# Exact exponentials of an attention kernel in a ring of three SBUF buffers instead of PSUM

## The reference

```python
def _attn_ref(q, k, v):
    B, H, S, D = q.shape                                   # 4, 8, 1152, 64
    scale = 1.0 / np.sqrt(D)
    q_pool = q.reshape(B, H, S // 2, 2, D).mean(axis=3)
    scores = scale * np.matmul(q_pool, k.transpose(0, 1, 3, 2))
    scores = scores - np.max(scores, axis=-1, keepdims=True)
    attn = np.exp(scores)
    attn = attn / (np.sum(attn, axis=-1, keepdims=True) + 1e-09)
    return np.matmul(attn, v).astype(np.float32)

def _moe_ref(x, w_in, w_out):                              # 512 -> 2048 -> 512
    h = x @ w_in
    return ((h * (1.0 / (1.0 + np.exp(-h)))) @ w_out).astype(np.float32)

def _moe2_ref(x, w1, w2, w3, w_out):                       # 512 -> 1024 -> 512
    return (((x @ w1) * (x @ w2)) @ w3 @ w_out).astype(np.float32)
```

## Time and profile before

| what | value |
|---|---|
| median of 3 runs | 1292.55 us (1292.16 to 1293.73) |
| the profiled execution | 1292.74 us, its span 1291.0 us |
| instructions | 26235 |
| TensorE busy | 1279.6 us, 99% |
| VectorE / ScalarE / GpSimd busy | 604.9 / 588.9 / 364.6 us |
| granted clock of TensorE | 1.00 |

### The profile page before, as it was taken

One profiled execution on the slowest core, in us unless ns is written; L12 is line 12 of the kernel. 1 busy time (PEld: TensorE's weight loads), 2 busy tenths in 40 slices (PEclk: granted clock), 3 DMA queues, 4 the chain that ended last, 5 costly groups with the idle time before them and its releaser, 6 DMA issues.

```text
span 1291.0 us, 26235 instructions
## 1 busy us (share of the span) xinstructions
PE 1279.6 (99%) x10980; PEld 1152.0 (89%) x10980; DVE 604.9 (47%) x904; ACT 588.9 (46%) x1081; POOL 364.6 (28%) x312
## 2 busy tenths in 40 slices
PE   8999999999999999999999999999999999999999
PEld 6999999999999999888888888888988888888888
DVE  6788788888887878443212111111156222222222
ACT  3777777777777776743322222222245212121111
POOL 4566766666666666510000000000000000000000
PEclk9999999999999999999999999999999999999999
DMA  4222222222222211021000000001052000000001
GB/s 141 66 69 64 71 75 74 75 74 75 75 74 74 75 56 38 20 67 49 17 1 1 1 1 1 1 1 49 2 180 98 1 1 34 1 33 1 33 5 46
DMA packets 26007, 58.60 MB, mean 45 GB/s; under 512 B 7200, under 2 KB 8736, under 8 KB 25888
## 3 DMA queue, kind: packets, MB, share of 16 engines
q1 hardware_dynamic: 25888, 56.91, 13.9%
HBM read 52.04 MB, written 4.79 MB: 44 GB/s over the span
## 4 chain that ended last, share of the span: by engine, by line
PE 97%; DVE 1%; POOL 0%; DMA 0%; issue 0%; ACT 0%; SPq 0%; POOLq 0%; DVEq 0%; ACTq 0%
PE psum L945 19%; PE psum L946 19%; PE psum L947 19%; PE psum L1021 18%; PE psum L962 10%; PE psum L998 9%; PE psum L1000 3%; DVE mx L734 1%; PE psum L973 1%; DMA kraw<-in_kT 0%; POOL pL L464 0%; POOL kL L450 0%; ACT pH L554 0%; PE psum L1031 0%; POOL qsum L492 0%
## 5 line engine op out<-in xcount | busy, mean ns | idle before, releaser
L734 DVE TENSOR_REDUCE mx<-psum 128x2 f32<-128x768 f32 x240 | 228.5, 957 | 72.0 <-PE psum L962 69.8
L554 ACT ACTIVATE pH<-psum 128x576 fp32r<-128x576 f32 x288 | 187.9, 653 | 145.6 <-PE psum L1000 142.7
L464 POOL TENSOR_TENSOR pL<-pF,pH 128x576 fp32r<-128x576 f32 x111 | 158.3, 1426 | 148.2 <-ACT pF L561 148.1
L876 DVE TENSOR_TENSOR gL<-gF,gH 128x512 fp32r<-128x512 f32 (+1 forms) x80 | 52.2, 653 | 310.3 <-ACT gH L636 310.3
L1021 PE MATMUL psum<-pH,vH 64*128 64x288 f32 x1152 | 187.9, 297 | 1.9 <-POOL pL L464 0.9
L1021 PE MATMUL psum<-pH,vL 64*128 64x288 f32 x1152 | 185.6, 292 | 0.0
L1021 PE MATMUL psum<-pL,vH 64*128 64x288 f32 x1152 | 185.4, 292 | 0.0
L633 ACT ACTIVATE gF<-psum 128x512 f32<-128x512 f32 (+1 forms) x80 | 44.4, 556 | 269.8 <-PE psum L947 269.8
L768 DVE TENSOR_TENSOR pL<-psum,pH 128x576 fp32r<-128x576 f32 x177 | 132.8, 750 | 35.1 <-ACT psum L563 35.1
L1021 PEld LDWEIGHTS psum<-pH,vH 64*128 64x128 f32 x1152 | 123.5, 185 | 4.4 <-POOL pL L464 1.6
L1021 PEld LDWEIGHTS psum<-pH,vL 64*128 64x128 f32 x1152 | 123.9, 185 | 0.0
(11 more groups left out here) (104 smaller groups left out, 2799.0 us busy)
## 6 DMA issues: line engine op xcount, KB each, us to landing
vraw<-in_v SPq DMA_DIRECT2D x16, 576.0 KB, 4.6
qraw<-in_qT SPq DMA_DIRECT2D x15, 576.0 KB, 5.0
kraw<-in_kT SPq DMA_DIRECT2D x15, 576.0 KB, 3.8
rsums<-recips SPq DMA_DIRECT2D x32, 144.0 KB, 3.1
wstage<-in_w_in SPq DMA_DIRECT2D x16, 256.0 KB, 4.6
fstage<-in_w3T SPq DMA_DIRECT2D x8, 512.0 KB, 4.7
w12stage<-in_w SPq DMA_DIRECT2D x8, 512.0 KB, 4.7
outT<-oS SPq DMA_DIRECT2D x4, 1024.0 KB, 4.2
```

The source lines that it names most:

```text
L464: pool.tensor_tensor(pL[r][:], pF[pool_order(n) % 2][:], pH[r][:].bitcast(F32), ALU.subtract).then_inc(pL_pool, 1)
L554: act.activation(pH[r][:], scores, ACT.Exp, scale=SCALE).then_inc(pH_ready, 1)
L734: dve.tensor_reduce(mx[:, qt, :, kb], bank[:, :, 0:KW], AX.X, ALU.max).then_inc(max_taken, 1)
L876: dve.tensor_tensor(gL[r][:, w], gF[:, w], gH[r][:, w].bitcast(F32), ALU.subtract).then_inc(gL_ready, 1)
```

## The change

`pF` becomes a ring of three buffers, used by all units: the exact exponential of unit n goes to `pF[n % 3]` and never back into `stbank`. VectorE's `p_lo` takes its first input from there. ScalarE waits, ahead of the exact exponential of n, for the low part of n - 3. TensorE's transposed scores of unit n wait for the exact exponential of n - 2, for every unit, where they waited for the low part of n - 2 for units of VectorE.

```diff
--- before.py
+++ after.py
@@ -112,7 +112,7 @@
             mrow = [sb(f"mrow{j}", [Q], F32R, st) for j in range(2)]
             vH = sb("vH", [NC, 3, D], F32R, st)
             vL = sb("vL", [NC, 3, D], F32R, st)
-            pF = [sb(f"pF{r}", [2, HALF], F32, st) for r in range(2)]
+            pF = [sb(f"pF{r}", [2, HALF], F32, st) for r in range(3)]
             pH = [sb(f"pH{r}", [2, HALF], F32R, st) for r in range(RING)]
             pL = [sb(f"pL{r}", [2, HALF], F32R, st) for r in range(RING)]
             mx = sb("mx", [QT, 2, KB], F32, st)
@@ -461,7 +461,7 @@
                 pool.wait_ge(pH_ready, n + 1)
                 need(pool, pv_done, 2 * (n - RING + 1))
                 r = n % RING
-                pool.tensor_tensor(pL[r][:], pF[pool_order(n) % 2][:], pH[r][:].bitcast(F32), ALU.subtract
+                pool.tensor_tensor(pL[r][:], pF[n % 3][:], pH[r][:].bitcast(F32), ALU.subtract
                                    ).then_inc(pL_pool, 1)
 
             def w_lo(i):
@@ -556,11 +556,9 @@
                     place_even(between)
                 if n % NC == 1 and n > NC:
                     take_o((n - NC) // UNITS, (n - NC) // NC % 2)
-                if by_pool(n):
-                    need(act, pL_pool, pool_order(n) - 1)
-                    act.activation(pF[pool_order(n) % 2][:], scores, ACT.Exp, scale=SCALE).then_inc(pF_ready, 1)
-                else:
-                    act.activation(scores, scores, ACT.Exp, scale=SCALE).then_inc(pF_ready, 1)
+                if n >= 3:
+                    act.wait_ge(*lo_done(n - 3))
+                act.activation(pF[n % 3][:], scores, ACT.Exp, scale=SCALE).then_inc(pF_ready, 1)
 
             def place_even(p):
 
@@ -765,7 +763,7 @@
                 dve.wait_ge(pF_ready, n + 1)
                 dve.wait_ge(pH_ready, n + 1)
                 need(dve, pv_done, 2 * (n - RING + 1))
-                dve.tensor_tensor(pL[r][:], stbank[n % 2], pH[r][:].bitcast(F32), ALU.subtract).then_inc(pL_dve, 1)
+                dve.tensor_tensor(pL[r][:], pF[n % 3][:], pH[r][:].bitcast(F32), ALU.subtract).then_inc(pL_dve, 1)
 
             def w_hi(i):
                 dve.wait_ge(wstage_loaded, 16 * (i + 1))
@@ -988,7 +986,7 @@
                     pe.wait_ge(m_placed_even, 2 * (p + 1))
                     pe.wait_ge(m_placed_odd, p + 1)
                 if n >= 2:
-                    pe.wait_ge(*((pF_ready, n - 1) if by_pool(n - 2) else lo_done(n - 2)))
+                    pe.wait_ge(pF_ready, n - 1)
                 keys, q = slice(c * P, (c + 1) * P), qhalf(a)
                 out = stbank[n % 2]
                 for s, (k, r) in enumerate(((kH, qH), (kL, qH), (kH, qL))):
```

## The result

The changed kernel takes 1348.93 us (median, 1348.46 to 1349.39), the kernel before 1292.22 us in the same comparison: a ratio of 1.0433, 95% interval 1.0423 to 1.0444, or 56.7 us more. Forecast were 1329 us, with a range of 1303 to 1356.

The account below looks back on a forecast made before the run. The bound was the slackless ring of TensorE's score block and VectorE's maximum. Holds of 37 us, less 0.2 for TensorE's wait, plus 0.5 for longer subtractions, on 1292.5 gave 1329 us, range 1303 to 1356.

Parts of the forecast that it names:

- TensorE's wait: Transposed scores of unit n wait for ScalarE's exponential of n-2, not the subtraction: 0.2 us gained, at most 1 us.
- ScalarE's wait: ScalarE's exact exponential of n waits for the low part of n-3; by program order it costs nothing.
- ScalarE's writes: 177 exponentials go to SBUF instead of PSUM, 654 ns for 651 each: nothing.
- The hold: VectorE's two-SBUF-input subtractions wait for a running GpSimd instruction and end 0.61 us after it.
- The sum over the holds of subtractions: Holds of VectorE's eleven subtractions laid over one old pair: 2.45 us a pair, 15 pairs, 37 us.
- the first item: VectorE's subtraction at 268.76, held by GpSimd's q sum until 270.17: next maximum 1.02 us late.
- The third: VectorE's subtraction at 281.38, held by GpSimd's normalizing product until 282.51: 0.68 us.
- GpSimd held by VectorE ... I take zero: Subtractions block GpSimd instructions up to 0.6 us, mostly hidden in its idle time: zero, up to 1 us a pair.
- Clock ... I take no change: TensorE's granted clock stays at 1.00, 2.4 GHz, though stalls make it idle 7% of the attention stage.
- no hold: Rival: VectorE's subtraction isn't held beside GpSimd and stays at 0.75 us; 1292 to 1294 us; chance 0.10.
- phases settle: Rival: VectorE's subtractions slide into GpSimd's idle time; 0.75 us a pair remain, 11 us, 1304 us; chance 0.13.
- the two engines fill up: Rival: held GpSimd work also stalls TensorE, 1 to 2 us a pair; 68 us and more, 1360; chance 0.12.

Follow-up runs that it names:

- the run with another order: Changed kernel with GpSimd's low part of k between its subtractions of units 15 and 16, not ahead of both: 1322.54 us, ratio 1.0228.
- 1316: Changed kernel with the reduced maxima (mcol) in unused columns of a PSUM bank: 1316.39 us, ratio 1.0179.
- 1308 us: Changed kernel with the maxima in PSUM and GpSimd's sum of q behind its subtraction of unit 7: 1307.68 us, ratio 1.0112.
- 1325: Kernel before, with VectorE's subtraction taking its first input from a constant tile of zeros in SBUF: 1325.33 us, ratio 1.0246.
- 1334: Changed kernel with GpSimd's low part of k behind its subtractions of units 15 and 16: 1333.56 us, ratio 1.0311.
- 1324 us: Changed kernel with maxima in PSUM, q's sum behind unit 7's subtraction, k's low part behind the subtractions of units 15 and 16: 1323.95 us, ratio 1.0238.
- the first two experiments: Changed kernel with VectorE's subtraction reading PSUM: 1292.73 us; kernel before with only that subtraction's first input moved to SBUF zeros: 1325.33 us.

## Where the prediction was right, and where its size came out by luck

**TensorE's wait, ScalarE's wait, ScalarE's writes: right.** With all of the change but the second SBUF input the time is 1292.73 us, and a fourth buffer changes nothing. ScalarE's two kinds of writes, 651 and 654 ns, are 653 ns for all. The waits in the trace have none of ScalarE for a subtraction. VectorE's own length stayed at 750 ns in the median, where 755 were forecast; it didn't get shorter either.

**The hold: right in kind.** 0.60 to 0.63 us from the end of GpSimd's instruction to that of the held subtraction, against the forecast 0.61; the longest is 2.02 us, near 2 as forecast, the mean 0.99 for about 1.1. The rule of the Trainium skill (SBUF — State Buffer, Who interferes with whom) covers it: two SBUF inputs on VectorE against GpSimd's reads. The trace of the changed kernel agrees, and so does the run whose only edit is that input (1017 ns in the mean for 750). Of the two kinds of instruction that the prediction counted as agreeing with that rule, only the negation has two SBUF inputs; the cast has one and shows only that it is held.

**The sum over the holds of subtractions: too large, 37 us for 23.** With the negation out of the way the loss is 1316.4 - 1293.2 = 23.2 us, 1.5 us a pair instead of 2.45 (in the trace a steady pair takes 34.95 us there for 33.25, which is 1.7); the low bound that I gave was 21. In the list, the first item was right in kind (the subtraction beside the sum of q ends 1.95 us after its start, 1.20 later than unheld; taking it away gave 8.7 us, 0.6 a pair, not 1.02). The third, 0.68 us, did not come: VectorE's subtraction of 270.71 started 0.02 us ahead of the normalizing product, and GpSimd was held. In its place the subtraction of unit 14 (274.62) was held 0.98 us, because GpSimd's subtraction of unit 13 ran late. And the cast of `w_hi`, 1062 ns in the median before, is mostly free in the changed kernel (498 ns in the mean). A list taken from the old timeline gives the size of such holds, not which instruction will be held.

**The step that failed: "GpSimd held by VectorE ... I take zero".** I looked for who waits for GpSimd's late results. What I didn't ask is what VectorE instruction a late GpSimd meets. Before, GpSimd's subtraction of unit 15 ran from 286.76 to 288.18 and the next began at 288.62, so the negation of 287.84 waited 0.2 us and found the gap. Holds of GpSimd ahead of them, about 1 us in all, closed that gap: the two ran back to back, and the negation, on TensorE's path, was held for 2.3 us in each of 13 pairs. (Back to back alone is not enough for so long a hold, as the run with another order shows.) TensorE waits 24.4 us for it, 0.9 of them in the first pair as before, so its cost is 23.5 us.

**The step "Clock ... I take no change": wrong.** The prediction named a lower clock among the signs of being wrong, and it came. Six pairs at the lower level for 3.4 us took 38.2 and not 36.8 us: 6 x 1.44 = 9 us. In the steady part it came only behind stalls of TensorE of 1.8 us: where those are gone (1316, 1322 and 1308 us, and 1325, 1334 and 1324 us) there is none. At the start it is otherwise: near 28 us the profiled executions of the changed kernel, of the one with a ring of four, of the one with the maxima in PSUM and of the one that subtracts from PSUM have one such stretch, behind an idle time of about 1.15 us that the kernel before has too, without it. The stretch from 500 to 552 of the earlier trace rows, with an idle share of 3.5%, was a poor witness, since its idle time came in short pieces (0.3 us at most).

Together: 23 for the subtractions, 23.5 for the negation and 9 for the clock are 55.5 of the 56.7 us; the rest is about what the medians of the kernel before differ by from one comparison to the other (1292.2 and 1293.2). The negation and its clock are the 32.5 us of one run; their split is read from the trace. The pair took 36.8 or 38.2 us and not 35.7. That the measured time lay in the range was luck: the first term was 14 us too high while two terms were missing. The term that I had, rightly sized, would have given 1316 us. Of the rivals, "no hold" is refuted by the first two experiments; "phases settle" is half true (the low bound of the subtractions); "the two engines fill up" came near in its size, but through the negation and not by TensorE waiting at L1019 for GpSimd's low parts, which is 1.6 us.

**Left open.** Why the negation lost to GpSimd's second subtraction in the changed kernel, each of 13 times, and won in the run with one SBUF input added to the kernel before and in the one with another order, with GpSimd's next instruction equally close behind. Neither the length of the instruction nor how early GpSimd's next is released tells the cases apart. Open too is why only six of the thirteen equal stalls were followed by the lower clock. What still costs 15 us in the kernel of 1307.68 us was seen in its timeline only (units 11 to 14 and 0 to 3) and not taken apart by runs.

## What to carry to other kernels

Ahead of moving an input of a VectorE instruction from PSUM to SBUF, count its SBUF inputs. With two of them it and the GpSimd instructions beside it, all of which read SBUF here, held each other up; with one it was never held (745 to 759 ns). What the move frees in PSUM has to be worth that. Look in the trace for a two-input instruction with a long maximum, and price the holds on both engines: a delayed instruction meets others that were safe before by a gap of half a microsecond. A short two-input instruction on the critical path can be freed of the holds by putting one small input into PSUM (2.3 us became 0.16, and the kernel 32.5 us faster).

## What the runs showed of the hardware

- A held VectorE subtraction of 576 columns ends 0.60 to 0.63 us after GpSimd's instruction (66 of them), where a free one takes 0.75: some 0.14 us of its start is spent inside the hold.
- A held VectorE subtraction came between two GpSimd instructions, and the second is recorded 0.5 us longer (q's low part 1.32 us for 0.81). A negation of 10 columns lost that turn in 13 of 13 cases in the changed kernel and waited for a second instruction of 1.4 us too (2.3 us for 0.16 of work), and got it in 13 of 13 in two other kernels (0.95 us).
- With starts 0.02 us apart the earlier instruction ran free and the later was held (VectorE at 270.71 took 0.74 us, GpSimd at 270.73 took 2.02 for 1.43).
- A subtraction with both inputs in SBUF and one with an input in PSUM take the same 750 ns at 576 columns.
- After six of thirteen stalls of 1.8 us TensorE was granted 1.2 GHz for about 3.4 us, which cost 1.44 us each. After the stalls of 0.9 to 1.3 us in the steady part of the other runs it wasn't, but once near the start it was, behind one of 1.15 us, in four of the profiled executions.
